# Another order of the token blocks: third block first, the first two last, and the first x in one transfer

## What is computed

```python
w = softmax(weight_gen)                    # over the 7 taps
x_pad = concatenate([zeros(B, 6, D), x])   # along the sequence
out[b, s, h] = sum_k w[b, s, h, k] * x_pad[b, s + k, h]
h = out.reshape(B * S, D) @ w_in           # 192 x 2048
g = s * maximum(h, 0) ** 2 + b
return g @ w_out                           # 2048 x 192
```

## Time and profile before

| | us |
|---|---|
| median of 3 runs | 1140.21 |
| lowest, highest | 1140.19, 1141.2 |
| the profiled execution | 1141.12 |
| its span | 1139.4 |
| PE busy in it | 1129.6 |

### The profile page before, as it was taken

The page is one execution under the profiler, slowest core; times in us unless marked ns, Lnnn a source line. Parts: engine busy times, 40 slices in busy tenths (PEclk is TensorE's granted clock), DMA queues, the critical chain, the costliest instruction groups (busy, mean ns, idle before and its releaser), DMA issues.

```text
span 1139.4 us, 31575 instructions
## 1 busy us (share of the span) xinstructions
PE 1129.6 (99%) x12956; PEld 1030.3 (90%) x12956; DVE 918.6 (81%) x1106; ACT 721.5 (63%) x746; POOL 123.1 (11%) x79
## 2 busy tenths in 40 slices
PE   8999999999999999999999999999999999999998
PEld 6999999999999999999999999999999999999997
DVE  8999887788877788877888777888778887778834
ACT  6776665566566666665665666566656666666663
POOL 2100111100111101111001111011110011110111
PEclk8999999999999999999999999999999999999999
DMA  9512334333244343343332442433433334424121
GB/s 254 92 54 61 86 91 118 87 94 102 76 108 117 69 112 80 89 117 87 95 93 80 113 117 65 116 77 92 117 81 100 84 86 116 117 65 116 35 59 29
DMA packets 97417, 106.73 MB, mean 94 GB/s; under 512 B 7187, under 2 KB 77730, under 8 KB 97390
## 3 DMA queue, kind: packets, MB, share of 16 engines
q1 hardware_dynamic: 94437, 103.61, 34.9%
q0 software_dynamic: 2512, 2.26, 1.3%
q10 hardware_dynamic: 440, 0.47, 0.2%
HBM read 70.63 MB, written 35.39 MB: 93 GB/s over the span
## 4 chain that ended last, share of the span: by engine, by line
PE 98%; DVE 1%; DMA 0%; ACT 0%; issue 0%; SPq 0%; DVEq 0%; ACTq 0%
PE hp L1033 47%; PE op L1071 35%; PE op L1078 16%; DMA x_in<-in_x 0%; PE op L949 0%; PE op L955 0%; SPq L231 0%; DVE scratch L810 0%; DVE scratch L806 0%; DVE g_lo L762 0%; ACT scratch L464 0%; ACT g_hi L471 0%; DVE wo L725 0%; DVE scratch L780 0%; ACT xT1s L438 0%
## 5 line engine op out<-in xcount | busy, mean ns | idle before, releaser
L1071 PE MATMUL op<-wo,g_hi 64*128 64x384 f32 x4096 | 594.3, 356 | 1.2 <-DVE g_lo L762 1.1
L1078 PE MATMUL op<-wo,g_lo 64*128 64x192 f32 x4096 | 514.3, 247 | 0.0
L460 ACT ACTIVATE scratch<-hp 128x1024 f32<-128x1024 f32 x254 | 255.7, 1019 | 376.3 <-PE hp L1033 374.3
L762 DVE TENSOR_TENSOR g_lo<-scratch,g_hi 128x1024 fp32r<-128x1024 f32 x255 | 324.1, 1272 | 186.5 <-ACT g_hi L471 182.3
L1078 PEld LDWEIGHTS op<-wo,g_lo 64*128 64x128 f32 x4096 | 392.5, 188 | 5.3
L1071 PEld LDWEIGHTS op<-wo,g_hi 64*128 64x128 f32 x4096 | 385.3, 184 | 7.2 <-issue 1.5
L1033 PE MATMUL hp<-xT1s,w_hi 64*128 64x512 f32 x2048 | 320.3, 390 | 0.5 <-ACT xT1s L438 0.3
L464 ACT ACTIVATE scratch<-scratch 128x1024 f32<-128x1024 f32 x255 | 269.9, 1059 | 6.0
L1033 PEld LDWEIGHTS hp<-xT1s,w_hi 64*128 64x128 f32 x2048 | 183.0, 185 | 33.9 <-issue 0.6
L1033 PE MATMUL hp<-xT1s,w_lo 64*128 64x512 f32 x1024 | 202.4, 391 | 0.0
L675 DVE TENSOR_TENSOR tap<-x_in,w_soft 128x768 f32<-128x768 f32 x186 | 177.5, 955 | 3.2
(11 more groups left out here) (74 smaller groups left out, 281.1 us busy)
## 6 DMA issues: line engine op xcount, KB each, us to landing
x_in<-in_x SPq DMA_DIRECT2D x30, 960.0 KB, 4.9
x_bounce<-x_parts SPq DMA_DIRECT2D x116, 192.0 KB, 3.4
xT1s<-x_bounce SPq DMA_DIRECT2D x29, 512.0 KB, 3.8
xT2s<-x_bounce SPq DMA_DIRECT2D x58, 256.0 KB, 4.9
out<-scratch SPq DMA_DIRECT2D x124, 96.0 KB, 1.8
w_in<-in_weight_gen SPq DMA_DIRECT2D x32, 112.0 KB, 2.1
wo_raw<-in_moe_w_out SPq DMA_DIRECT2D x4, 384.0 KB, 7.4
wo_sums<-in_moe_w_out POOLq DMA_DIRECT2D x4, 384.0 KB, 6.9
```

Of the source, the lines that this page charges most:

```text
L460: nc.scalar.activation(r[:, b, :], hp[:, PAIR * b:PAIR * (b + 1), :], ACT.Relu).then_inc(relu_done, 1)
L762: nc.vector.tensor_tensor(g_lo[:, buf, tiles, :], pair, g_hi[:, buf, tiles, :].bitcast(F32), ALU.subtract).then_inc(g_lo_ready, 1)
L1071: nc.tensor.matmul(op[:, t, 0:2 * D], g_hi[rows[h], g % 2, j, t * P:(t + 1) * P], wo[rows[h], k, :, :].rearrange("p a d -> p (a d)"), star ...
L1078: mm = nc.tensor.matmul(op[:, t, 0:D], g_lo[rows[h], g % 2, j, t * P:(t + 1) * P], wo[rows[h], k, 0, :], start=False, stop=(k == FT - 1 an ...
```

## The change

Step i now takes block i + 2 (`AHEAD = 2`) for i from 0 to 29, step 30 takes block 0 and step 31 block 1. So steps 0 and 1 have no halo, and each loads its x with one `load_x`. Blocks 0 and 1 are loaded by `edge_loads` near the end: for each batch one transfer of the halo with 31 rows and one of zeros, from a new tile `zeros` that POOL clears; SP then waits until these eight have landed, and issues the main transfer, on whose semaphore alone DVE waits. The halo issues of ACT and SP at the start go, with the memsets of x_in on DVE and POOL. In the first step the tap of which ACT makes a half is tap 1 instead of tap 0; tap 0 is whole on DVE. Stores follow the new order.

```diff
+    AHEAD = 2
+    ACT_TOK, ACT_TAP = 2, 1
...
-    last_quarter_rows = quarter_rows[:, :, (STEPS - 1) * STEP * D:STEPS * STEP * D]
+    last_block = AHEAD - 1
+    last_quarter_rows = quarter_rows[:, :, last_block * STEP * D:(last_block + 1) * STEP * D]
...
+        zeros = sb("zeros", [B, PAD * D])
...
+            def load_edge_x(block):
+
+                missing = PAD - STEP * block
+                sp.wait_ge(zeros_ready, 1)
+                for q in range(B):
+                    a = q * batch_rows
+                    sp.dma_start(x_in[a + 1:a + batch_rows, block, 0:missing, :],
+                                 x_rows[a:a + batch_rows - 1, (TOK - missing) * row:TOK * row]).then_inc(x_edge_loaded[block], FETCH)
+                    sp.dma_start(x_in[a:a + 1, block, 0:missing, :].rearrange("p t d -> p (t d)"),
+                                 zeros[q:q + 1, 0:missing * row]).then_inc(x_edge_loaded[block], FETCH)
+                sp.wait_ge(x_edge_loaded[block], 2 * B * FETCH)
+                sp.dma_start(x_in[:, block, missing:, :], x_rows[:, 0:STEP * (block + 1) * row]).then_inc(x_loaded[block], FETCH)
...
-            load_w(0)
-            load_first_x(0)
-            load_halo(sp, 0, first_halves)
+            load_w(AHEAD)
+            load_x(AHEAD, 0)
             load_w1(0)
...
-            load_first_x(1)
-            load_halo(sp, 1, ((1, 120), (121, 7)))
+            load_x(1 + AHEAD, 1)
...
+            def edge_loads(i, block):
+                sp.wait_ge(w_shifted, i + 2)
+                load_w(block)
+                sp.wait_ge(tap_ready, K * (i + 1))
+                load_edge_x(block)
...
-            loads(STEPS - 4, 0)
+            edge_loads(STEPS - 4, 0)
             bounce(STEPS - 3, 1)
             store(STEPS - 5)
-            loads(STEPS - 3, 1)
+            edge_loads(STEPS - 3, 1)
             bounce(STEPS - 2, 0)
             store(STEPS - 4)
             bounce(STEPS - 1, 1)
             store(STEPS - 3)
-            store(STEPS - 2)
+            store(STEPS - 2, 0)
...
-            for q in range(PAIR):
-                zero_batch_start(nc.gpsimd, 0, q).then_inc(pool_zeroed, 1)
-                pool.wait_ge(pool_zeroed, q + 1)
...
+            nc.gpsimd.memset(zeros[:, :], 0.0).then_inc(zeros_ready, 1)
...
-            pool.wait_ge(x_halo_loaded[1], 2 * FETCH)
-            for q in range(B):
-                zero_batch_start(nc.gpsimd, 1, q).then_inc(pool_zeroed, 1)
-                pool.wait_ge(pool_zeroed, PAIR + q + 1)
...
-            load_halo(act, 0, second_halves)
-
...
-                products(K - 1, 0, STEP).then_inc(tap_ready, 1)
-                products(K - 2, 1, STEP - 1)
-                dve.wait_ge(x_halo_loaded[0], 2 * B * FETCH)
-                dve.wait_ge(pool_zeroed, PAIR)
-                dve.wait_ge(dve_zeroed, B - PAIR)
-                products(K - 2, 0, 1).then_inc(tap_ready, 1)
-                for k in reversed(range(1, K - 2)):
-                    products(k, 0, STEP).then_inc(tap_ready, 1)
-                products(0, 0, STEP - ACT_TOK).then_inc(tap_ready, 1)
+                for k in reversed(range(K)):
+                    products(k, 0, STEP - ACT_TOK if k == ACT_TAP else STEP).then_inc(tap_ready, 1)
...
-            for q in range(PAIR, B):
-                zero_batch_start(nc.vector, 0, q).then_inc(dve_zeroed, 1)
...
-                if k == 0:
+                if k == ACT_TAP:
                     pe.wait_ge(act_tap_ready, 1)
```

More of the change, by code:

```diff
@@ L53, in mix_and_mlp @@
     EPS = 1e-9
-    ACT_TOK = 2
+    AHEAD = 2
+    ACT_TOK, ACT_TAP = 2, 1
     WARM_UP = 4
@@ L131, in mix_and_mlp @@
         x_loaded = [sem("x_loaded_even"), sem("x_loaded_odd")]
-        x_halo_loaded = [sem("x_halo_loaded0"), sem("x_halo_loaded1")]
+        x_edge_loaded = [sem("x_edge_loaded0"), sem("x_edge_loaded1")]
         w_loaded = sem("w_loaded")
@@ L141, in mix_and_mlp @@
         ident_ready = sem("ident_ready")
-        pool_zeroed = sem("pool_zeroed")
-        dve_zeroed = sem("dve_zeroed")
+        zeros_ready = sem("zeros_ready")
         w1_hi_ready = sem("w1_hi_ready")
@@ L224, in by_token @@
             return rows.rearrange("p (u e h c) -> p u e h c", u=STEP // 2, e=2, h=2)[:, :, e, :, :]
[L226 to L232, removed]
         def store_last(queue, n, t):
@@ L238, in mix_and_mlp @@
         batch_rows = S // TOK
[L239 to L246, removed]
         @block.sync
@@ L252, in _, with load_w, load_x @@
             wcol = STEP * H * K
-            def load_w(i):
-                sp.dma_start(w_in[:, :, :], w_rows[:, bass.ds(i * wcol, wcol)]).then_inc(w_loaded, FETCH)
-            def load_x(i, parity):
+            def load_w(block):
+                sp.dma_start(w_in[:, :, :], w_rows[:, bass.ds(block * wcol, wcol)]).then_inc(w_loaded, FETCH)
+            def load_x(block, parity):
                 sp.dma_start(x_in[:, parity, :, :],
-                             x_rows[:, bass.ds((i * STEP - PAD) * row, (STEP + PAD) * row)]
+                             x_rows[:, bass.ds((block * STEP - PAD) * row, (STEP + PAD) * row)]
                              ).then_inc(x_loaded[parity], FETCH)
-            def load_first_x(i):
-                before = PAD - STEP * i
-                sp.dma_start(x_in[:, i, before:, :], x_rows[:, 0:(STEP * (i + 1)) * row]).then_inc(x_loaded[i], FETCH)
+            def load_edge_x(block):
[9 more added lines that the diff above has]
+                sp.dma_start(x_in[:, block, missing:, :], x_rows[:, 0:STEP * (block + 1) * row]).then_inc(x_loaded[block], FETCH)
             def load_w1(g):
@@ L278, in store_by_token, with store @@
             def store_by_token(i):
+                block = i + AHEAD
                 sp.wait_ge(out_ready, i + 1)
                 for t in range(STEP):
-                    sp.dma_start(out_rows[:, (i * STEP + t) * row:(i * STEP + t + 1) * row], out_sb[:, t, :]).then_inc(out_stored, FETCH)
-            def store(i):
+                    sp.dma_start(out_rows[:, (block * STEP + t) * row:(block * STEP + t + 1) * row], out_sb[:, t, :]).then_inc(out_stored, FETCH)
+            def store(i, block=None):
                 sp.wait_ge(out_ready, i + 1)
+                block = i + AHEAD if block is None else block
                 for t in range(STEP):
-                    sp.dma_start(quarter_rows[:, :, bass.ds(i * (STEP * row) + t * row, row)],
+                    sp.dma_start(quarter_rows[:, :, bass.ds(block * (STEP * row) + t * row, row)],
                                  out_sb[t * Q:(t + 1) * Q, :, :]).then_inc(out_stored, FETCH)
@@ L312, in _ @@
             sp.wait_ge(w_shifted, 1)
-            load_w(1)
+            load_w(1 + AHEAD)
             load_w1(1)
             load_w1(2)
-            load_first_x(1)
-            load_halo(sp, 1, ((1, 120), (121, 7)))
+            load_x(1 + AHEAD, 1)
             load_wo(2)
@@ L326, in loads @@
                 sp.wait_ge(w_shifted, i + 2)
-                load_w(i + 2)
+                load_w(i + 2 + AHEAD)
                 sp.wait_ge(tap_ready, K * (i + 1))
-                load_x(i + 2, parity)
+                load_x(i + 2 + AHEAD, parity)
+            def edge_loads(i, block):
[3 more added lines that the diff above has]
+                load_edge_x(block)
             loads(0, 0)
@@ L374, in _ @@
                                     base=0, pattern=[[-1, P]], channel_multiplier=1).then_inc(ident_ready, 1)
-            pool.wait_ge(ident_ready, 1)
+            nc.gpsimd.memset(zeros[:, :], 0.0).then_inc(zeros_ready, 1)
             def sum_wo(c):
@@ L581, in first_products @@
                 act.wait_ge(w_soft_ready, 1)
-                act.wait_ge(x_halo_loaded[0], 2 * B * FETCH)
-                act.wait_ge(pool_zeroed, PAIR)
-                act.wait_ge(dve_zeroed, B - PAIR)
+                act.wait_ge(x_loaded[0], FETCH)
                 for t in range(STEP - ACT_TOK, STEP):
                     for h in range(H):
-                        last = nc.scalar.activation(first_taps[:, 0, t, h * G:(h + 1) * G], x_in[:, 0, t, h * G:(h + 1) * G], ACT.Copy,
-                                                    scale=w_soft[:, t, h, 0:1])
+                        last = nc.scalar.activation(first_taps[:, ACT_TAP, t, h * G:(h + 1) * G],
+                                                    x_in[:, 0, ACT_TAP + t, h * G:(h + 1) * G], ACT.Copy,
+                                                    scale=w_soft[:, t, h, ACT_TAP:ACT_TAP + 1])
                 last.then_inc(act_tap_ready, 1)
@@ L644, in products, with taps @@
                         ALU.mult)
-                products(K - 1, 0, STEP).then_inc(tap_ready, 1)
-                products(K - 2, 1, STEP - 1)
-                dve.wait_ge(x_halo_loaded[0], 2 * B * FETCH)
-                dve.wait_ge(pool_zeroed, PAIR)
-                dve.wait_ge(dve_zeroed, B - PAIR)
-                products(K - 2, 0, 1).then_inc(tap_ready, 1)
-                for k in reversed(range(1, K - 2)):
```

(17 more changed lines are left out.)

## The result

| | before | changed |
|---|---|---|
| median, us | 1140.2 (6 runs) | 1145.38 (6 runs) |
| lowest to highest | 1139.92 to 1141.2 | 1144.72 to 1146.14 |
| profiled execution, its span | 1141.12, 1139.4 | 1144.82, 1143.0 |

The ratio is 1.0044, 95% interval 1.0033 to 1.0055: slower by 5.2 us at the medians, where 3.7 (1143.9) was forecast. The two profiled executions are 3.7 us apart (3.6 in span).

A forecast was written before the change was run, and what follows sets the result against it. PE was taken as the bound, busy 1129.6 of 1139.4 us. Profiled 1141.12 - 0.6 (start) + 2.6 (stall) + 1.7 (clock) = 1144.8, or 1143.9 for the median; range 1139.5 to 1147.5.

The forecast's parts named there:

- How the 31 rows are shared out: Edge loads: 31 is prime, so each halo transfer runs on one DMA engine at 25.9 GB/s, 22.1 us for four.
- main x issued, after the first halo issue: SP's queue near the end: 1.7 us plus 22.1 us for halos issued from 992.67, landed at 1016.5.
- bounce late by: SP's queue behind the halo wait: the bounce starts at 1016.95 instead of 1008.73, 8.2 us late.
- stall of PE: PE near 1025 to 1028: waits 1.5 us for xT1s, works 0.7, waits 1.2 for xT2s, in all +2.6.
- clock behind it: PE after the stall: 6.8 us at half clock would cost 3.4, no fall nothing; middle taken, +1.7.
- start: First 15 us: x in one transfer lands at 6.4, first product at 14.06, gain 0.4 to 0.8, taken as -0.6.
- its end of -1.5: Start, best case: x lands at 6.0, the clock does not fall, DVE ends last, product starts at about 13.3.
- The case without a fall of the clock: Rival after the edge-load stall: PE stands still 2.6 us, then runs at full rate, 1142.2; chance 0.33.
- Spread halos: Rival at the edge loads: rows or halos spread over engines, bounce on time, only the start left, 1139.6; chance 0.14.
- A slow engine: Rival at the edge loads: one engine runs at 13 GB/s, stall of 24 us, time 1165; chance 0.05.
- a late start: Rival at the start: x lands at 8.7, costing 1.5 instead of gaining 0.6, time 1146.0; chance 0.05.
- Covered terms: Near the end: step 30's x lands about 1019.2, costing DVE nothing; second edge load hidden by 6 us.

The follow-up runs named there:

- Experiment 1: Changed kernel with each batch's halo in two transfers of 16 and 15 rows instead of one of 31; median 1139.76, ratio 0.9992 to the kernel before.
- experiment 3: Changed kernel with one of block 0's four halos split into 16 and 15 rows, the other three at 31; median 1139.57, ratio 0.9995 to the kernel before.
- experiment 2: Changed kernel without SP's wait for the 31-row halos, DVE waiting for them instead; median 1141.43, ratio 1.0005 to the kernel before.
- experiment 5: Changed kernel with two rounds of unused warm-up matmuls on PE at the head of step 29; median 1144.51, 3.92 us over the kernel before.

## Why the prediction was right

**The direction and the place** held: a stall at step 29, behind a bounce behind the halo of block 0, and nowhere else. The measured 1145.38 lies 1.5 above the forecast.

**How the 31 rows are shared out** was inferred from packet counts (15, and 15 + 7) and holds: 26 GB/s on 6.6% of the engines against the 25.9 of the estimate. The trace agrees with the rule of the Trainium skill, "DMA: Bandwidth & Descriptors", section "Why a DMA increments its semaphore by 16 and not by 1", also in that the four transfers share one engine: between 998 and 1013 us the rate stays at one engine's worth. Experiment 1 shows that the loss comes from this, experiment 3 that it has a threshold, and experiment 2 that the one engine's ring, and not only the program's wait, stands in the way.

**The sizes**, term by term for the profiled execution:

| term | forecast | measured |
|---|---|---|
| main x issued, after the first halo issue | 23.8 | 24.6 |
| bounce late by | 8.2 | 9.0 |
| stall of PE | +2.6 | +3.6 |
| clock behind it | +1.7 | +1.7 |
| start | -0.6 | -1.7 |
| sum | +3.7 | +3.6 |

The stall was forecast a microsecond too small, and 0.8 of it is the time from the first halo issue to the main x. The halo rows themselves were sized well: their large packets run without a break to speak of from 992.7 to 1015.0, 22.3 us where 22.1 was forecast. What the prediction had too small is what comes beside the bytes, 1.7 us: the first row moved 1.6 us after its issue, and SP issued the main x another 0.7 us after the last. The issues that became slow (below) did not cost this time. While SP sat in the last of them (996.32 to 1000.88) the engine had no break, as the transfers between 997 and 1000 us show:

```profile
DMA packets 20, 0.08 MB, mean 26 GB/s; under 512 B 3, under 2 KB 3, under 8 KB 20
...
q1 hardware_dynamic: 20, 0.08, 6.4%
```

The clock fell, but for 3.4 us of full work, not for 6.8; the middle of the bounds met it by luck. The prediction read the fall at the old start off PE's low activity from 5 to 7 us. That sign does not decide: the changed kernel had less there (0.41 of 2.00 us against 0.78), with the same pause of 1.87 us before the first sum, and its clock stayed full. So the start gained more in this execution: DVE, not PE, ended last, the case that the prediction had as its end of -1.5.

So the sum is right for this pair of executions partly by two errors that cancel, a stall 1.0 too small and a start 1.1 too small. At the medians they don't. Experiment 1 has the new start without the stall; the changed kernel is 5.6 over it, so the end cost 5.6 where 4.3 (2.6 + 1.7) was forecast, and the start gained 0.9 where 0.6 was. Before itself is some 0.5 slower in the larger sample (1140.69) than the 1140.21 that the forecast started from. 1.3 - 0.3 + 0.5 is the 1.5 by which the forecast was low. The term that was mis-sized is the end, and within it the stall. The profile shows 5.3 of its 5.6 us. (Each taken against its own before, the end is 5.2 + 0.9 = 6.1; the 0.5 between the two is the difference of the samples of before.) The mean granted clock was 0.998, 0.998 and 0.996 in the three shorter executions of the changed kernel and 0.996, 0.996 and 0.995 in the three longer (1145.79 to 1146.14), which fits a clock that was low for longer there, but these have no profile.

**The rivals.** The case without a fall of the clock is what experiment 5 made: a stall of 3.8. Spread halos are experiment 1; the prediction gave them 1139.6, measured 1139.76. A slow engine and a late start did not occur: x landed 4.79 us after its issue, not 5.1.

**Covered terms.** DVE waited 1.7 us for the x of step 30, within its idle time. The second edge load issued its main x at 1038.60, and the next bounce followed at 1047.20: hidden, as forecast.

## What to carry to other kernels

Before a transfer is merged or moved, look at the number of its rows: one of 31 rows ran on a single engine at 26 GB/s, and cutting it into 16 and 15 rows, with more issues, took 5.6 us off the kernel (1145.38 to 1139.76). Then ask who stands behind it: a hand-written queue passes a delay on only once the next item's slack is used up (4.5 us late cost nothing, 9.0 cost 3.6 and the clock), so the slack is to be read from the trace before anything slow is put in front of it. And split a first load by order of use, in large pieces.

## What was not expected of the hardware

- Issuing itself slowed down behind the 31-row transfers. The third and fourth zero transfer took SP 2.17 and 4.56 us to issue instead of 0.6, and in experiment 2 the four issues of the bounce took 6.75 instead of 2.61. Block 1's four transfers of 31 rows, whose rows are a third as long (1536 bytes), had no slow issue: the zero transfers between them took 0.50 to 0.56. A full ring would explain it; it was not measured by itself.
- Two waits of PE, 1.74 and 1.44 us with 0.9 of work between, were followed by a half clock (1.2 GHz) for 3.4 us of full work; waits of 0.80 and 1.19 with the same work between, behind 1.5 us of unused matmuls, were not (experiment 5).
- At the start of the same kernel the clock fell in one profiled execution and not in another: experiment 5 and the changed kernel are the same there, and were at 0.50 and 1.00 around 10 to 13 us. In experiment 5 x landed later, and DVE began at 6.72 us instead of 6.18; whether that made the difference is not shown.
